# Chunk 5's scores from stacked keys and queries in an mLSTM layer with two gated feed-forward layers

## The chip, the cores and the metric

One core of one Trainium2 chip. The metric is the device time of one execution in microseconds (us), the median of three runs. The profile is of one further execution.

## The reference

Three stages follow each other, all in float32.

```python
# 1: mLSTM attention, B=2, H=8, S=768, D=40; for each t:
m_new = maximum(f[t] + m, i[t])
C = exp(f[t]+m-m_new) * C + exp(i[t]-m_new) * outer(v[t], k[t])
n = exp(f[t]+m-m_new) * n + exp(i[t]-m_new) * k[t]
y[t] = sigmoid(o[t]) * (C @ q[t]) / maximum(abs(n @ q[t]), 1)
# 2: x = y as [1536, 320];  x = (sigmoid(x @ w_gate) * (x @ w_val)) @ w_out     (d_ff = 1536)
# 3:                        x = ((x @ w_a) * (x @ w_b)) @ w_out2                (d_ff = 1536)
```

## The kernel before, in words

**Tiling.** The attention is done in 12 chunks of 128 steps; chunk n is batch n % 2 and time block n // 2. The feed-forward layers work on three groups of 512 tokens (4 chunks) and 12 tiles of 128 hidden columns. One pass of one tile over one group is a unit, and there are 72 units in all. A unit's `up` (line 558) makes 16 matmuls of 512 columns, 8 for the gate and 8 for the value, from the weights' high and low parts, and `down` (L580) makes 12 matmuls of 320 columns.

**Interleaving.** Chunks 0 to 3 come first. Chunk 4 is begun ahead of unit 0, and from there on one chunk goes with three units: `piece(u)` (L79) gives chunk n and step k of unit u. Unit 0 is (4, 1), unit 1 is (4, 2), unit 2 is (5, 0), unit 3 is (5, 1), unit 4 is (5, 2), unit 5 is (6, 0) and so on. On TensorE (L640 to L661) the scores of chunk n stand between the two halves of `up` in the unit with k = 1, and its values behind `down` of the unit before. In the unit with k = 2 the state matmuls stand between the halves, and `turn(n)` (L515), which transposes the chunk's finished output `x_n`, stands ahead of `down(u - 1)`. So whatever holds up a turn holds up all of TensorE's program.

**Scores, two ways.** `scores` (L438) has two forms. Below `STACKED` it is 4 matmuls of float32 keys `k3` against a block-diagonal `q_blk` (L472), and the trace shows each as two instructions. From `STACKED` on it is 8 matmuls, one to a head, of `stack[0]` against `stack[1]` (L463). A stack holds a head's 40 rows three times over in its 120 partitions, as high and low parts in float32r. `load_both` (L297) brings keys (to `k_both`) and queries (to `q_blk[0]`) from DRAM, three times each, in 12 transfers of 120 or 40 KB, 960 KB in all. ScalarE's `part_high` (L689) copies each with a sign by row to the stack, and VectorE's `stack_low` (L933) adds the rest. These stand in the unit with k = 2 ahead of the chunk: on ScalarE ahead of the copy of the turned output and of the two weight tiles' copies (L823 to L836), on VectorE behind `h_low` and ahead of `x_low` (L1052 to L1056).

**Weights.** Each weight tile of 544 KB comes by `load_w(j)` (L334) to a ring of three `w_raw`; ScalarE's `w_high(j)` (L701) makes the high part, GpSimd's `w_low(j)` (L1110) the low part. `load_w(j)` waits until tile j - 3 has been through both. `up(u, 0)` of the first group waits for `w_low` of its tile.

**Other work on the way to a turn.** SyncE's `load_o(4)` (L329) brings chunk 4's output gate. In unit 0 ScalarE's program is `gate(0)`, `w_high(2)`, `open_gate(4)` (L696, the sigmoid of the output gate), `h_high(0)`. VectorE's is `hidden(0)`, `h_low(0)`, then in unit 1 `combine(4)` (L891), `state(4)`, `hidden(1)`. GpSimd's is `decay(4)`, `open_x(4)` (L1077, two multiplications that give `x_n`), `mask(5)`, `w_low(3)`. All these queues run strictly in program order, and the order is written out by hand.

SyncE's program just ahead of the loop, and the guard of its transfers:

```python
load_w(2)
sp.wait_ge(dve_gate, 20)
store_rows(m_row, a_dram, 2, CHUNKS, st_rows)
load_w(3)
load_o(4)
load_w(4)
...
wait(sp, dve_stack, 2 * (n - STACKED))                    # load_both(n)
wait(sp, pe_s, 2 * n if n == STACKED and x else 0)        # x = 1: the queries
```

Of the kernel before, what the change touches and what calls it, by code (L numbers as in the profile page):

```python
# [43 lines left out]
UNITS = 2 * NG * NF  # L44
ALONE = 4
RING = 3
STACKED = 6
LOW = -1.0e30
BIG = 2.0 ** 100
HI, LO = 0, 32  # L50
# [2 lines left out]
def wait(eng, sem, value):  # L53

    if value > 0:
        eng.wait_ge(sem, value)


def set_of(n):

    return n % 2 if n < ALONE else 0
# [17 lines left out]
def piece(u):  # L79

    n, k = divmod(u + 1, 3)
    n += ALONE
    return (n, k) if n < NCH else (None, None)
# [7 lines left out]
def build(nc, f_in, i_in, q_in, kq3_in, vk_in, o_in, w1_in, w2_in, consts_in, bm_in, out):  # L91
    ctx = ExitStack()
    with ctx:
# [172 lines left out]
        def _(sp):  # L266
            def load_rows(n):

                s = set_of(n)
                if n > ALONE:  # L270
                    sp.wait_ge(act_e, 2 * n)
                else:
                    wait(sp, pe_ab, 2 * before(n) + 2)
                if n > ALONE:
                    sp.dma_start(levels[s][:, :],
                                 a_dram[n * HEADS * P:(n + 1) * HEADS * P].partition_broadcast(P)).then_inc(ld_a[s], 16)
                    return
                for at, tile in ((HI, a_hi), (LO, a_lo))[:1 if n < BATCH else 2]:
                    sp.dma_start(arow[s][at:at + 1, :].bitcast(F32), row_source(tile, n)).then_inc(ld_a[s], 16)

            def load_k(n):

                s = set_of(n)
                wait(sp, pe_s, 2 * before(n) + 2)
                sp.dma_start(k3[s][:, :], kq3_in[n, :, 0:3 * P]).then_inc(ld_q[s], 16)

            def load_q(n):

                s = set_of(n)
                if n >= BATCH:  # L290
                    load_k(n)
                for j, k in ((0, 3), (1, 3), (2, 2)):
                    own = slice(j * HD, (j + 1) * HD)
                    sp.dma_start(q_blk[s][own, 3 * j * P:(3 * j + k) * P],
                                 kq3_in[n, own, 3 * P:(3 + k) * P]).then_inc(ld_q[s], 16)

            def load_both(n):  # L297

                wait(sp, dve_stack, 2 * (n - STACKED))
                for x in range(2):  # L300
                    wait(sp, pe_s, 2 * n if n == STACKED and x else 0)
                    for r in range(3):
                        own = both[x][r * HD:(r + 1) * HD, :]
                        sp.dma_start(own[:, 0:6 * P].rearrange("d (j c) -> d j c", j=2),
                                     kq3_in[n, 0:2 * HD, 3 * x * P:3 * (x + 1) * P]
                                     .rearrange("(j d) c -> d j c", j=2)).then_inc(ld_both[x], 16)
                        sp.dma_start(own[:, 6 * P:], kq3_in[n, 2 * HD:, 3 * x * P:(3 * x + 2) * P]
                                     ).then_inc(ld_both[x], 16)

            def load_v(n):  # L310

                s = set_of(n)
                wait(sp, pe_fv, before(n) + 1)
                wait(sp, pe_t, before(n) + 1 if last_with_state(before(n)) else 0)
                sp.dma_start(vk[s][:, :], vk_in[n]).then_inc(ld_v[s], 16)

            def load_scaled(n):

                s = set_of(n)
                wait(sp, pe_f, before(n) - 1)  # L320
                sp.dma_start(q3[s][:, :], kq3_in[n, :, 3 * P:6 * P]).then_inc(ld_i[s], 16)
                rows = i_dram[n * HEADS * P:(n + 1) * HEADS * P].rearrange("(h t) -> h t", t=P)
                for j in range(3):
                    src = rows[j::3, :].unsqueeze(0)
                    k = src.shape[1]
                    sp.dma_start(i_rep[s][j * HD:(j + 1) * HD, 0:k * P].rearrange("d (x t) -> d x t", t=P),
                                 src.to_broadcast([HD, k, P])).then_inc(ld_i[s], 16)

            def load_o(n):  # L329

                wait(sp, pool_x, n if n > ALONE else 0)
                sp.dma_start(osig_b[n % 2][:, :], o_in[:, n * DM:(n + 1) * DM]).then_inc(ld_o[n % 2], 16)

            def load_w(j):  # L334

                wait(sp, act_whi, j - RING + 1)
                wait(sp, pool_wlo, j - RING + 1)
                sp.dma_start(w_raw[j % RING][:, :], (w1_in, w2_in)[j // NF][j % NF]).then_inc(ld_w[j % RING], 16)

            def store_rows(tile, dst, c0, c1, done):  # L340

                sp.dma_start(dst.rearrange("(c r t) -> r c t", r=ROWS, t=P)[:, c0:c1, :],
                             tile[:, c0 * P:c1 * P].rearrange("r (c t) -> r c t", t=P)).then_inc(done, 16)
# [42 lines left out]
            load_w(2)  # L386
            sp.wait_ge(dve_gate, 20)
            store_rows(m_row, a_dram, 2, CHUNKS, st_rows)
            load_w(3)
            load_o(4)  # L390
            load_w(4)
# [2 lines left out]
            for u in range(3 * (NCH - ALONE) - 2):  # L394
                n, k = piece(u)
                if k == 0 and n > ALONE:
                    load_o(n)
                if k == 1 and n + 1 < NCH:
                    load_rows(n + 1)
                    if n + 1 < STACKED:  # L400
                        load_q(n + 1)
                    elif n + 1 == STACKED:
                        load_both(n + 1)
                if k == 0 and STACKED <= n < NCH - 1:
                    load_both(n + 1)
                if k == 2 and n + 1 < NCH:
                    load_scaled(n + 1)
                    load_v(n + 1)
                if u + 5 < NF:
                    load_w(u + 5)  # L410
# [13 lines left out]
        def _(pe):  # L424
# [13 lines left out]
            def scores(n, half):  # L438

                s = set_of(n)  # L440
                if n >= STACKED:
                    wait(pe, dve_stack, 2 * (n - STACKED) + 2)
# [814 lines left out]
```

## Time and profile before

| what | value |
|---|---|
| median of three runs | 467.82 us (467.71 to 467.88) |
| the profiled execution's own time | 467.95 us |
| its span | 466.1 us |
| TensorE busy | 459.0 us |
| VectorE, ScalarE, GpSimd busy | 197.9, 197.5, 114.2 us |
| moved by the transfers | 37.42 MB |

The span is what the profiler saw from the first to the last instruction; the execution's own time holds 1.85 us besides. In the rows below a timeline line gives the start (us from the span's start), the length, the engine, the kernel's line, the operation, what it writes and reads, and in brackets how long the engine stood idle before it and what released it. In the chain of work that ended last a line gives start, length and the work. PE is TensorE, DVE VectorE, ACT ScalarE, POOL GpSimd and SPq the SyncE queue that issues transfers.

### The profile page before, as it was taken

The page shows a single profiled execution, that of the slowest core. Times are in us where ns is not written, and L with a number is a line of the kernel's source. Part 1 is how long each engine was busy: PE and PEld are TensorE (multiplying, and loading weights), DVE is VectorE, ACT ScalarE, POOL GpSimd, SP SyncE. Part 2 cuts the span into 40 slices and gives each one's busy share as a digit, 9 for nine tenths or more (in the row PEclk, how much of TensorE's full clock was granted, in tenths as well). Part 3 has the DMA queues.
Part 4 walks back from the last instruction along what each step waited for, and adds up shares of the span by engine and source line. Part 5 has one row for each costly group of instructions (what it writes and reads, how often), then busy time and mean ns, then how long its engine had stood idle before and what let it go on. Part 6 is the DMA issues. An engine that isn't in the chain of part 4 may idle for free.

```text
span 466.1 us, 6631 instructions
## 1 busy us (share of the span) xinstructions
PE 459.0 (98%) x2527; PEld 403.6 (87%) x2527; DVE 197.9 (42%) x352; ACT 197.5 (42%) x360; POOL 114.2 (25%) x110
## 2 busy tenths in 40 slices
PE   8999999999999999999999999999999999999997
PEld 5888898898989899888888888888888888888886
DVE  8778366746564645334222243222322222322223
ACT  5964838566482836233434452222222222222222
POOL 4488757643213020002445540000000000000000
DMA  5887686352534460000332300000010000100001
GB/s 156 219 271 220 206 248 183 124 155 76 135 110 139 113 203 35 1 2 13 128 99 97 96 1 0 0 2 0 9 49 1 0 1 0 58 0 1 0 1 56
DMA packets 21449, 37.42 MB, mean 80 GB/s; under 512 B 2835, under 2 KB 15670, under 8 KB 21418
## 3 DMA queue, kind: packets, MB, share of 16 engines
q1 hardware_dynamic: 21050, 35.94, 25.4%
q10 hardware_dynamic: 208, 0.71, 0.5%
q8 instruction: 20, 0.33, 0.3%
q0 software_dynamic: 160, 0.35, 0.3%
q14 instruction: 11, 0.09, 0.1%
HBM read 34.91 MB, written 2.04 MB: 79 GB/s over the span
## 4 chain that ended last, share of the span: by engine, by line
PE 86%; DVE 5%; ACT 3%; issue 2%; POOL 2%; DMA 2%; SPq 1%; ACTq 0%; DVEq 0%; POOLq 0%
PE bank L575 53%; PE bank L592 26%; PE bank L497 3%; DMA w_raw<-w_in 1%; ACT pt L680 1%; PE bank L488 1%; PE bank L463 1%; PE bank L553 1%; PE bank L523 1%; DVE h_lo L955 1%; POOL cst L1100 1%; POOL x_n L1085 1%; DVE pt L886 1%; DMA f_row<-f_in 1%; DVE sign L1036 1%
## 5 line engine op out<-in xcount | busy, mean ns | idle before, releaser
L949 DVE TENSOR_TENSOR h_ff<-bank,s_ff 128x512 f32<-128x512 f32 x72 | 49.8, 691 | 173.2 <-PE bank L575 173.0
L575 PE MATMUL bank<-xt,w_hi 128*128 128x512 f32 x360 | 118.7, 395 | 0.0
L744 ACT CAST h_hi<-h_ff 128x512 fp32r<-128x512 f32 x72 | 44.6, 619 | 126.5 <-DVE h_ff L949 123.5
L737 ACT ACTIVATE s_ff<-bank 128x512 f32<-128x512 f32 x72 | 43.1, 598 | 126.0 <-PE bank L575 125.6
L575 PE MATMUL bank<-xt,w_lo 128*128 128x512 f32 x216 | 84.4, 391 | 0.0
L955 DVE TENSOR_TENSOR h_lo<-h_ff,h_hi 128x512 fp32r<-128x512 f32 x72 | 59.6, 828 | 57.3 <-ACT h_hi L744 57.3
L575 PEld LDWEIGHTS bank<-xt,w_hi 128*128 128x128 f32 x360 | 65.5, 188 | 12.0 <-DVE t_st L923 0.4
L575 PE MATMUL bank<-xt,w_hi_mid 128*128 128x512 f32 x180 | 59.2, 394 | 0.0
L575 PE MATMUL bank<-xt,w_hi_end 128*128 128x512 f32 x180 | 59.1, 393 | 0.0
L575 PEld LDWEIGHTS bank<-xt,w_lo 128*128 128x128 f32 x216 | 40.6, 188 | 8.8
L592 PE MATMUL bank<-w_hi,h_hi 128*128 128x320 f32 x144 | 45.3, 314 | 0.2 <-DVE h_lo L955 0.2
L592 PE MATMUL bank<-w_lo,h_hi 128*128 128x320 f32 x144 | 44.4, 308 | 0.0
L592 PE MATMUL bank<-w_hi,h_lo 128*128 128x320 f32 x144 | 44.4, 308 | 0.0
L575 PE MATMUL bank<-xt,w_lo_end 128*128 128x512 f32 x108 | 42.2, 391 | 0.0
L575 PE MATMUL bank<-xt,w_lo_mid 128*128 128x512 f32 x108 | 42.2, 391 | 0.0
L1114 POOL TENSOR_TENSOR w_lo<-w_raw,w_hi 128x1088 fp32r<-128x1088 f32 (+1 forms) x12 | 29.8, 2484 | 45.9 <-ACT w_hi L716 45.9
L575 PEld LDWEIGHTS bank<-xt,w_hi_end 128*128 128x128 f32 x180 | 32.9, 188 | 5.8
L575 PEld LDWEIGHTS bank<-xt,w_hi_mid 128*128 128x128 f32 x180 | 32.8, 188 | 5.7
L592 PEld LDWEIGHTS bank<-w_hi,h_hi 128*128 128x128 f32 x144 | 27.1, 188 | 1.6 <-DVE h_lo L955 0.6
L592 PEld LDWEIGHTS bank<-w_lo,h_hi 128*128 128x128 f32 x144 | 27.1, 188 | 1.2
L592 PEld LDWEIGHTS bank<-w_hi,h_lo 128*128 128x128 f32 x144 | 27.0, 188 | 0.0
L575 PEld LDWEIGHTS bank<-xt,w_lo_mid 128*128 128x128 f32 x108 | 20.3, 188 | 4.4
(125 smaller groups left out, 677.9 us busy)
## 6 DMA issues: line engine op xcount, KB each, us to landing
w_raw<-w_in SPq DMA_DIRECT2D x24, 544.0 KB, 4.0
vk<-vk_in SPq DMA_DIRECT2D x12, 344.0 KB, 3.4
levels<-a_scratch SPq DMA_DIRECT2D x7, 512.0 KB
k_both<-kq_in SPq DMA_DIRECT2D x18, 120.0 KB
q_blk<-kq_in SPq DMA_DIRECT2D x18, 120.0 KB
y<-rows_t SPq DMA_DIRECT2D x12, 160.0 KB, 1.9
q<-kq_in SPq DMA_DIRECT2D x10, 180.0 KB
osig_b<-o_in SPq DMA_DIRECT2D x8, 160.0 KB, 3.0
```

The lines of the kernel that those rows point to most:

```text
L463: mm = pe.matmul(st[:, h * P:(h + 1) * P], stack[0][:, own], stack[1][:, own], start=True, stop=True)
L488: mm = pe.matmul(acc[:, h * VW:(h + k) * VW], q3[s][:, x * P:(x + 1) * P], cst[p][:, h * VW:(h + k) * VW], start=(x == 0), stop=False)
L497: mm = pe.matmul(acc[:, h * VW:(h + 1) * VW], pt[s][:, h * P:(h + 1) * P], vk[s][:, h * VW:(h + 1) * VW], start=(n < BATCH and h == 0), st ...
L523: mm = pe.transpose(tp[:, j * P:(j + 1) * P], x_n[s][:, j * P:(j + 1) * P], ident[:, :])
L553: mm = pe.transpose(tp[:, j * P:(j + 1) * P], rows_t[tb][:, j * P:(j + 1) * P], ident[:, :])
L575: mm = pe.matmul(up_bank(u, gv)[:, :], w_part(low, f, (gv * 3 + kt) * P, P), xt[:, xb * TOK + g * TG:xb * TOK + (g + 1) * TG], start=(j == ...
L592: mm = pe.matmul(OB[tb][:, 0:DM], h[r][:, tb * P:(tb + 1) * P], w_part(low, f, W1C, DM), start=(f == 0 and j == 0), stop=(f == NF - 1 and ...
L737: act.activation(s_ff[u % 2][:, :], up_bank(u, 0)[:, :], ACT.Sigmoid if u < UNITS // 2 else ACT.Copy).then_inc(act_s, 1)
L744: act.copy(h_hi[u % 2][:, :], h_ff[u % 2][:, :]).then_inc(act_h, 1)
L949: dve.tensor_tensor(h_ff[u % 2][:, :], up_bank(u, 1)[:, :], s_ff[u % 2][:, :], ALU.mult).then_inc(dve_h, 1)
L955: dve.tensor_tensor(h_lo[u % 2][:, :], h_ff[u % 2][:, :], h_hi[u % 2][:, :].bitcast(F32), ALU.subtract).then_inc(dve_hlo, 1)
L1114: pool.tensor_tensor(w_part(1, j % NF, at, WC - at), w_raw[j % RING][:, at:], w_part(0, j % NF, at, WC - at).bitcast(F32), ALU.subtract).t ...
```

## The change

`STACKED` goes from 6 to 5, so chunk 5's scores are computed in the stacked form. Its `load_both` no longer stands in the loop; it is issued once ahead of `load_w(3)`. Within unit 1 its two copies (ScalarE) and two sums (VectorE) are new, by the loop's own conditions. In unit 0 the plain loads of chunk 5 (`load_q(5)`, one transfer of keys and three of queries, 340 KB) are gone, and `load_both(6)` moves from unit 3 to unit 2.

```diff
-STACKED = 6
+STACKED = 5
...
             store_rows(m_row, a_dram, 2, CHUNKS, st_rows)
+            load_both(STACKED)
             load_w(3)
             load_o(4)
             load_w(4)
...
                 if k == 1 and n + 1 < NCH:
                     load_rows(n + 1)
-                    if n + 1 < STACKED:
-                        load_q(n + 1)
-                    elif n + 1 == STACKED:
-                        load_both(n + 1)
                 if k == 0 and STACKED <= n < NCH - 1:
                     load_both(n + 1)
```

## Rows read from the trace of the kernel before

**Rows 1.** The page: busy time of TensorE, and VectorE's group of line 955.

```profile
PE 459.0 (98%) x2527; PEld 403.6 (87%) x2527; DVE 197.9 (42%) x352; ACT 197.5 (42%) x360; POOL 114.2 (25%) x110
...
L955 DVE TENSOR_TENSOR h_lo<-h_ff,h_hi 128x512 fp32r<-128x512 f32 x72 | 59.6, 828 | 57.3 <-ACT h_hi L744 57.3
```

**Rows 2.** The waits of TensorE from 30 us to the end: total, times, longest.

```profile
PE bank L523 <- POOL x_n L1085: 1.4, 3, 0.8
```

**Rows 3.** The chain that ended last, 50 to 60 us (unit 3).

```profile
52.35 1.84 PE bank L575 x8
54.20 1.73 PE bank L472 x8
55.93 1.85 PE bank L575 x8
```

**Rows 4.** The same chain, 94 to 101 us (unit 9).

```profile
97.42 0.85 PE bank L463 x8
98.26 1.90 PE bank L575 x8
```

**Rows 5.** Timeline of SyncE's queue ahead of and within unit 0.

```profile
30.54 0.42 SPq L342 DMA_DIRECT2D a_scratch<-m_row  x1
32.62 0.33 SPq L338 DMA_DIRECT2D w_raw<-w_in  x1
32.99 0.43 SPq L332 DMA_DIRECT2D osig_b<-o_in  x1
38.68 0.33 SPq L338 DMA_DIRECT2D w_raw<-w_in  x1
```

**Rows 6.** Timeline of SyncE's queue in unit 5: first issue of load_both(7), and the one behind.

```profile
71.29 0.30 SPq L304 DMA_DIRECT2D k_both<-kq_in  x1
...
75.91 0.35 SPq L338 DMA_DIRECT2D w_raw<-w_in  x1
```

**Rows 7.** The chain that ended last, 70 to 90 us.

```profile
75.91 5.04 DMA w_raw<-w_in
```

**Rows 8.** Tile osig_b, 20 to 95 us: issue to landing of its transfers.

```profile
DMA to landing us min/median/max: 2.3/4.1/6.7
```

**Rows 9.** Busy time by engine, 31 to 36 us, with clock, DMA share, GB/s last.

```profile
31.00:36.00 5.00, 4.98 (x25) 3.83 (x26) 4.13 (x9) 4.15 (x7) 5.00 (x6) 1.00 0.91 319
```

**Rows 10.** Timeline of ScalarE in units 0 and 1.

```profile
37.54 0.47 ACT L699 ACTIVATE osig_b<-osig_b 128x320 f32<-128x320 f32 x1 [0.75 <-DMA osig_b<-o_in]
...
39.26 0.62 ACT L744 CAST h_hi<-h_ff 128x512 fp32r<-128x512 f32 x1 [1.25 <-DVE h_ff L949]
...
45.58 2.11 ACT L716 CAST w_hi<-w_raw 128x1088 fp32r<-128x1088 f32 x2
```

**Rows 11.** Lines 694 and 936: shortest, middle and longest in ns, all six chunks.

```profile
L694 ACT ACTIVATE k_stack<-k_both,sign x6: 1146/1149/1151, 67.6 to 171.9; 120x1024 fp32r<-120x1024 f32 x6
```

```profile
L936 DVE SCALAR_TENSOR_TENSOR k_stack<-k_both,low_rows,k_stack x6: 1284/1285/1286, 68.8 to 173.1; 120x1024 fp32r<-120x1024 f32 x6
```

**Rows 12.** Timeline of VectorE in unit 0.

```profile
36.16 2.47 DVE L1036 TENSOR_SCALAR sign<-low_rows 120x2 f32<-120x2 f32 x1
...
39.91 1.72 DVE L955 TENSOR_TENSOR h_lo<-h_ff,h_hi 128x512 fp32r<-128x512 f32 x1 [0.69 <-ACT h_hi L744]
```

**Rows 13.** Timeline of GpSimd, units 0 to 4.

```profile
35.84 5.24 POOL L1114 TENSOR_TENSOR w_lo<-w_raw,w_hi 128x1088 fp32r<-128x1088 f32 x2
...
43.45 1.12 POOL L1085 TENSOR_TENSOR x_n<-x_raw,osig_b 128x320 f32<-128x320 f32 x1
...
46.77 2.54 POOL L1114 TENSOR_TENSOR w_lo<-w_raw,w_hi 128x1088 fp32r<-128x1088 f32 x1 [0.89 <-ACT w_hi L716]
...
63.66 0.86 POOL L1085 TENSOR_TENSOR x_n<-x_raw,osig_b 128x320 f32<-128x320 f32 x1
```

**Rows 14.** Timeline of TensorE: the turns of chunks 4 and 5.

```profile
44.62 0.55 PE L523 MATMUL bank<-ident,x_n 128*128 128x128 f32 x3 [0.77 <-POOL x_n L1085]
...
66.16 0.49 PE L523 MATMUL bank<-ident,x_n 128*128 128x128 f32 x3
```

## The prediction

> **What bounds the kernel now.** I read the page first. TensorE is busy for 98% of the span, and no other engine for more than 42% [rows 1]. Its waits came next: from 30 us to the end it stands still for its turns alone, 1.4 us in three waits, each for GpSimd's `x_n` [rows 2]. So any TensorE time saved behind 30 us comes off the end, and any lateness of another engine counts only where it reaches TensorE. The timelines then show where the margins are thin. Chunk 4's turn already comes late by 0.77 us [rows 14], so that chain has no slack at all.
>
> **Removed: the plain scores of chunk 5.** In unit 3 the eight plain instructions hold the chain for 1.73 us, with 1.85 us for the half of `up` behind them [rows 3]. In unit 9, of the same make-up, the eight stacked ones take 0.85 us, with 1.90 behind them [rows 4]. The saving is (1.73 + 1.85) - (0.85 + 1.90) = 0.83 us. Nothing hides TensorE, so all of it counts, unless a new stall eats it. `load_q(5)` goes too, four issues in unit 0 behind `load_w(4)`; nothing waited for them, so I take nothing for that.
>
> **Added: 12 issues on SyncE ahead of `load_w(3)`.** In unit 5 the same 12 begin at 71.29 and the issue behind them at 75.91 [rows 6], which is 4.62 us. SyncE is free from 30.54 + 0.42 = 30.96 and idles until 32.62, so part of the block fits in a gap [rows 5]. The queries wait for chunk 4's scores, the last TensorE work ahead of unit 0; they should be through at about the time (33.3) at which the six key issues are, so I price that wait at nothing. Then `load_w(3)` is issued at 30.96 + 4.62 = 35.6 and not 32.62, `load_o(4)` at 36.0 and not 32.99. Both are 3.0 us later. `load_w(4)` waits for GpSimd in any case and goes out at 38.68 [rows 5]: no change.
>
> **Who waits for these two.** Tile 3 is read by ScalarE at 45.58 only [rows 10], and by 41 it has landed: hidden. The gate is another matter. ScalarE's `open_gate(4)` already sat idle 0.75 us for it and began at 37.54, 4.55 us after the issue [rows 5, 10]. Three estimates give its new landing. The same 4.55 from 36.0 gives 40.55. The bytes ahead of it give the same: at 319 GB/s, with the transfers' engines 91% busy in that stretch [rows 9], 960 KB cost 3.0 us. A weight tile issued right behind this very block took 5.04 us to land [rows 7], so tile 3 would land at 40.65 and the gate some 0.4 us behind it, at 41.1. The shortest landing of this tile is 2.3 us and the longest 6.7 [rows 8], so the bounds are 38.3 and 42.7. I take 40.6, where two of the estimates agree.
>
> **What the late gate does.** Behind `open_gate(4)` on ScalarE stands `h_high(0)`, and behind that on VectorE `h_low(0)`, `combine(4)`, and on GpSimd `open_x(4)`, for which the turn waits. `h_high(0)` began at 39.26 [rows 10]. Now it begins at 40.6 + 0.4 = 41.0 and ends at 41.6. `h_low(0)` then starts at 41.65. It took 1.72 us before, from 39.91 to 41.63, beside GpSimd's two weight tiles that ran until 41.08 [rows 12, 13]. Now it starts behind them and takes about the group's mean of 0.83 [rows 1], so it ends at 42.5, later by 0.85. From there to the end of `x_n` at 44.57 [rows 13] the chain is unchanged, perhaps 0.1 shorter for less company. Chunk 4's turn comes 0.75 us later, a stall of 0.77 + 0.75 = 1.5. If the gate lands at 38.3, ScalarE has it before `h_high(0)` could start and nothing is lost; if at 42.7, the turn comes 2.1 us later than in my estimate, so the term lies between 0 and +2.9.
>
> **Moved in unit 1: two copies on ScalarE, two sums on VectorE.** The copies are 1.15 us each and overlap a little, 2.2 us together; the sums are 1.28 each [rows 11]. Their data are in by 39 to 40, well ahead. On ScalarE they stand ahead of `w_high(3)`, which began at 45.58 [rows 10], while `w_low(3)` ended at 46.77 + 2.54 = 49.31 [rows 13] and unit 3 began at 52.35 [rows 3]: a slack of 3.0 us. Against it stand 2.2 us of copies and about 1.2 of lateness that VectorE passes on through `hidden(1)`, while TensorE itself is later by 0.75. That leaves 0.4 us: just hidden. The sums end before `hidden(2)` is due, and `x_low(4)` is not read before the second group.
>
> **Further on in units 2 to 4.** ScalarE stays some 2 us late through the exponentials of chunk 5 and the copies of tiles 5 and 6; GpSimd's low parts of these stand ahead of `decay(5)` and `open_x(5)`. The latter ended at 63.66 + 0.86 = 64.52, with its turn at 66.16 [rows 13, 14], a slack of 1.64. By then TensorE stands at 66.16 - 0.83 + 0.75, about 66.1, and `x_n` is ready at about 66.4 to 66.5. I take a new stall of 0.3 us, between 0 and 0.8. Then the idle of all three engines absorbs the lateness. `load_both(6)` moves to unit 2, where it delays `load_w(7)` and the levels of chunk 6 by some 4 us, against more than that of slack; `load_both(7)` waits for chunk 6's sums as before, so the later stalls [rows 2] remain.
>
> **The sum.** -0.83 + 0.75 + 0.3 = +0.2 us, on the profiled execution's 467.95: 468.15. That execution was 0.13 us above the median of the runs, so against the median it is 468.0. A measurement of this kernel can tell about 0.2%, 0.94 us, from no change.
>
> **One rule of the skill weighed.** What the rows show: `sign`, a 120x2 operation, took 2.47 us, and `h_low(0)` 1.72, each ending just behind a GpSimd weight tile [rows 12, 13]. The Trainium skill (SBUF — State Buffer, "SBUF: two separate sides") says that VectorE and GpSimd share one pair of ports as an exclusive lock for a whole instruction; the trace agrees, by these two durations. By that rule the lateness in unit 2 can grow, which is the second rival below.
>
> **Rival 1: the loads are hidden.** If the gate lands by 39, ScalarE's `h_high(0)` isn't moved and the saving stands alone: 467.82 - 0.83 = 467.0. For it: the shortest landing of 2.3 us. Against it: ScalarE already waited for this transfer with 3 us more to spare. It is still within 0.2%. Chance 0.19, and 0.07 more that a stall shrinks as well and it falls below 466.9.
>
> **Rival 2: slower, through GpSimd's low parts.** `w_low(3)` now falls where VectorE has the added sums and `h_low(2)`, and `w_low(4)` where `h_low(2)` is due. If VectorE must sit out one tile more (2.5 us [rows 13]) or GpSimd one sum more (1.3 us [rows 11]), the slack of 0.4 in front of unit 3 becomes a stall of 0.9 to 2.1, and the turn of chunk 5 slips with it. The time would be 468.0 + 1.3 or so, 469.3 (468.9 to 470.1). It decides as soon as ScalarE's tile 3 copy ends later than about 50.4 (52.35 + 0.75 less 2.54 and a tenth). For it: two thin margins in a row. Against it: in the later chunks, where the same copies and sums stand, TensorE lost little. Chance 0.16. Beside this the gate could land at 42 or later, which gives 469.5 to 470 by the same turn; chance 0.06.
>
> **How the numbers follow.** The forecast (a new stall that about cancels the saving) has 0.52: 467.2 to 468.75. Faster by over 0.2% gets 0.07, slower 0.22, within it 0.71. The range runs from 466.9 to 469.5: the low end is the bare saving, the high end the middle of the slower cases, with about 2 in 10 outside.
>
> **What would show it.** Right: unit 3's scores take 0.85 us; `load_w(3)` is issued near 35.6; ScalarE's idle ahead of `open_gate(4)` grows to near 4 us; chunk 4's turn waits 1.5 us and not 0.77. Wrong: that turn still waits 0.8 us (rival 1), or a wait of `up` for `w_lo` appears ahead of unit 3 or TensorE's wait for chunk 5's turn is over 1 us (rival 2).

## The result and the profile after

| | before | changed |
|---|---|---|
| median | 467.85 us (467.71 to 469.89, 4 runs) | 475.21 us (474.82 to 476.55, 4 runs) |
| profiled execution: own time, span | 467.95, 466.1 us | 476.55, 474.8 us |
| mean granted clock of TensorE | 1.0 | 0.987 |

The ratio is 1.014 (95% interval 1.0104 to 1.0176): 7.4 us slower, where 468.0 (466.9 to 469.5) was forecast. The profiled execution is the longest of the four, 1.3 us above their median. In the changed kernel every line number behind line 400 is 3 lower, so line 575 is now 572.

The waits of TensorE, longest first, in the changed kernel:

```profile
PE bank L520 <- POOL x_n L1082: 7.5, 3, 6.9
```

It is the wait of [rows 2], and it has grown from 1.4 to 7.5 us, 6.9 of it at one place. The chain that ended last, from 36 to 66 us, tells which place and why:

```profile
36.65 0.35 SPq L338
...
37.05 8.86 DMA osig_b<-o_in
...
45.93 0.48 ACT osig_b L696
...
49.45 1.13 POOL x_n L1082
...
50.62 0.90 PE bank L520 x3
51.53 3.20 PE bank L589 x12
54.73 4.63 PE bank L572 x16
59.36 1.76 PE bank L589 x12
61.12 1.84 PE bank L572 x8
62.96 0.85 PE bank L460 x8
63.81 1.90 PE bank L572 x8
```

Chunk 4's output gate is issued at 37.05 and takes 8.86 us to land. ScalarE's sigmoid begins at 45.93 and not 37.54 [rows 10], and chunk 4's turn at 50.62 and not 44.62 [rows 14]. Then look at TensorE's own lengths: the first `down` behind the wait takes 3.20 us, the next one 1.76, for the same 12 matmuls. At the end stand the stacked scores, 0.85 us and not 1.73 [rows 3]. The busy time in stretches of 4 us shows both causes (TensorE's, its loads', VectorE's, ScalarE's and GpSimd's busy time with counts, then the clock, the transfer engines' share, GB/s):

```profile
36.00:40.00 4.00, 4.00 (x31) 3.71 (x30) 3.38 (x3) 1.10 (x1) 4.00 (x3) 1.00 0.91 201
40.00:44.00 4.00, 3.75 (x20) 2.86 (x18) 0.00 (x0) 0.00 (x0) 1.95 (x2) 1.00 1.03 224
44.00:48.00 4.00, 0.00 (x0) 0.00 (x0) 0.99 (x4) 1.47 (x3) 0.00 (x0) 0.81 1.02 375
48.00:52.00 4.00, 1.38 (x6) 1.38 (x7) 3.17 (x6) 1.52 (x2) 2.46 (x3) 0.50 0.49 149
52.00:56.00 4.00, 4.00 (x15) 3.71 (x14) 3.29 (x5) 3.56 (x5) 1.36 (x1) 0.50 0.00 0
56.00:60.00 4.00, 4.00 (x20) 3.37 (x19) 0.60 (x1) 2.39 (x4) 4.00 (x4) 0.91 0.40 135
60.00:64.00 4.00, 4.00 (x26) 3.62 (x25) 1.29 (x3) 3.97 (x10) 1.33 (x1) 1.00 0.75 226
```

From 36 to 44 us the transfer engines are full, yet they bring only 201 and 224 GB/s, against 319 in [rows 9]. And the granted clock, 1.00 until TensorE stopped at about 43.7, is 0.50 from 48 to 56: the lower of its two levels, 1.2 GHz, also for the first matmuls after the wait.

**Where the time went.** The stretch ahead of unit 0 changes from execution to execution (32.4 to 42.6 us in the profiles of this study; in the long ones TensorE's clock is at 0.50 for much of it, also in a variant of the kernel before), so from here on I count from the first matmul of unit 0 (32.88 us in the kernel before, 32.80 in the changed one) to the end of the span.

| stretch (us from unit 0's first matmul) | before | changed | difference |
|---|---|---|---|
| to chunk 4's turn | 11.74 | 17.82 | +6.08 |
| turn to chunk 5's scores | 9.41 | 12.18 | +2.77 |
| scores to the `down` behind them | 3.59 | 2.74 | -0.85 |
| on to the last `down` | 400.20 | 400.23 | +0.03 |
| last `down` to the end | 8.28 | 9.03 | +0.75 |
| sum | 433.22 | 442.00 | +8.78 |

The spans are read to 0.1 us, so the last two rows are good to about 0.05. The +0.75 at the end was no part of any theory. SyncE's wait for the last stores tells it, 1.5 us in the kernel before and 2.2 in the changed one:

```profile
SPq L93 <- DMA y<-rows_t: 1.5, 1, 1.5
```

```profile
SPq L93 <- DMA y<-rows_t: 2.2, 1, 2.2
```

### The profile page after: what moved, and what is told of

It is laid out like the page before. It is cut to its first block, busy times and chain, and to the rows that moved or that the text cites. A ratio compares the mean times of both kernels' runs of the same rounds, so it can differ in the third digit from the quotient of the medians.

```text
span 474.8 us, 6645 instructions
## 1 busy us (share of the span) xinstructions
PE 461.2 (97%) x2527; PEld 405.7 (85%) x2527; DVE 196.6 (41%) x354; ACT 199.1 (42%) x362; POOL 113.7 (24%) x110
## 4 chain that ended last, share of the span: by engine, by line
PE 85%; DMA 3%; DVE 3%; ACT 3%; SPq 2%; issue 2%; POOL 1%; ACTq 0%; DVEq 0%
PE bank L572 52%; PE bank L589 26%; PE bank L494 3%; DMA osig_b<-o_in 2%; DMA w_raw<-w_in 1%; PE bank L460 1%; ACT pt L677 1%; SPq L304 1%; SPq L307 1%; PE bank L485 1%; PE bank L550 1%; PE bank L520 1%; PE bank L508 1%; DMA f_row<-f_in 1%; DVE pt L883 0%
## 5 line engine op out<-in xcount | busy, mean ns | idle before, releaser
L952 DVE TENSOR_TENSOR h_lo<-h_ff,h_hi 128x512 fp32r<-128x512 f32 x72 | 55.3, 768 | 64.3 <-ACT h_hi L741 64.3
```

The lines of the kernel that those rows point to most:

```text
L952: dve.tensor_tensor(h_lo[u % 2][:, :], h_ff[u % 2][:, :], h_hi[u % 2][:, :].bitcast(F32), ALU.subtract).then_inc(dve_hlo, 1)
```

## The experiments

The chips that these ran on scattered more: the kernel before gave 467.3 to 477.5 us, with medians of 468.5 to 469.5. A ratio of whole times then has an interval of some 0.3% either way, so most verdicts rest on the stretches of the profiled executions, counted as above. That is one execution of each kernel, and they differ: the changed kernel took 442.00 us from unit 0 on in one profile and 438.49 in another (e12 below). Where the timed runs say something else than the profile, it is said.

### What stands ahead of the gate

**e1_gate_first:**

```diff
-            load_both(STACKED)
-            load_w(3)
             load_o(4)
+            load_both(STACKED)
+            load_w(3)
             load_w(4)
```

> Chunk 5's 12 transfers stay ahead of weight tile 3, but the output gate's transfer goes ahead of them. Theory A (the 7 us are the gate's late landing and what follows from it): the gate lands by 37.5 us or so, the turn of chunk 4 waits 1 us or less, TensorE's clock stays at full speed, and the time is the kernel before less 0.83 us plus at most 1 us: 467.0 to 468.0. Theory B (the added copies and sums in unit 1, or tile 3 behind 960 KB, are the loss): still over 470, with a wait for w_lo or w_hi ahead of unit 3.

Measured: the gate was no longer waited for, chunk 4's turn came at 11.72 and the clock stayed at 1.0. At the last `down` the kernel was ahead of the kernel before by 0.86 us, and at the end of the span by 0.08: 433.14 against 433.22. Ratio 1.0018 (0.9991 to 1.0046). Its turn wait, of the whole execution:

```profile
PE bank L520 <- POOL x_n L1082: 1.4, 3, 0.7
```

Theory B falls here. The copies, the sums and a tile 3 behind 960 KB are all still in this kernel, and in this execution not one of them stops TensorE.

**e2_block_behind:**

```diff
-            load_both(STACKED)
             load_w(3)
             load_o(4)
+            load_both(STACKED)
             load_w(4)
```

> The 12 transfers go behind tile 3 and the gate and ahead of tile 4, into the stretch in which the transfers stood still in the kernel before (36 to 39 us). Theory A: nothing that is waited for stands behind them; the gate lands at 37.5 as before, tile 4 and the levels are not late, and the bare saving is left: 467.0, between 466.8 and 467.5. Theory B (copies and sums cost): 468 to 469 by a stall in units 1 to 4.

Measured: turn at 11.74 with a wait of 0.77, as in [rows 14]; 0.79 us ahead from unit 3 to the last `down`, and 433.14 at the end. Ratio 1.0009 (0.9982 to 1.0036). The saving is real and is carried through all of the feed-forward work; 0.72 us of it go at the very end (below).

**e3_keys_ahead** (`load_both` in two halves: the keys where the change has it, the queries behind `load_o(4)`):

```diff
-            load_both(STACKED)
+            load_both(STACKED, (0,))
             load_w(3)
             load_o(4)
+            load_both(STACKED, (1,))
```

> Half the dose: the six transfers of the keys (480 KB) stay ahead of tile 3 and the gate, the six of the queries go behind them. If the lateness grows with what stands ahead, the gate lands between the kernel before (37.5) and the changed one (45.9): near 40 if it is the issues and bytes alone, and the turn of chunk 4 waits 1 to 2 us with the clock at full speed, 467.5 to 468.5. If the clock falls even so, 470 or more.

Measured: the gate took 6.9 us from issue to use. In the profiled execution it was issued early against TensorE's work (unit 0 began at 37.16), and the turn waited only 0.89 us. Behind it the clock stayed at 1.00, and from unit 0 on it took 433.14 us, no more than the kernel before. Over the timed runs the median was 472.76, ratio 1.0059 (1.0029 to 1.009), with a clock of 0.978 to 0.996 in each of the eight runs above 471. That half the dose stops TensorE at the turn in many of these is likely but not shown: the profiled execution is one of the eight, and its low clock lay ahead of unit 0 (0.50 from 30 to 34 us). What is shown is that the gate's landing grows with what stands ahead of it, and by more than I priced.

**e6_issues_only** (12 transfers of 4 bytes in place of the block, the real block behind the gate):

```diff
-            load_both(STACKED)
+            for i in range(12):
+                sp.dma_start(tiny[:, i:i + 1], kq3_in[5, 0:1, i:i + 1]).then_inc(ld_extra, 16)
             load_w(3)
             load_o(4)
+            load_both(STACKED)
```

> Twelve transfers of 4 bytes each stand ahead of tile 3 and the gate, chunk 5's real ones behind the gate. It is the lateness of the issue alone, some 4 to 5 us of queue without bytes: by my working the gate lands near 40.5 and the turn waits 1.5 us; 467.8 to 468.5. If small issues cost more than that it is seen as SyncE's gaps.

Measured: issued 2.1 us later against unit 0, the gate was used 3.6 us after its issue, and the turn waited 0.74 us. The waits in that execution:

```profile
PE bank L525 <- POOL x_n L1087: 1.5, 3, 0.7
```

So the late issue by itself costs nothing at the turn; without the block's bytes the gate even lands sooner behind its issue than the 4.55 us of the kernel before. The timed median was 469.83, ratio 1.0007 (0.9981 to 1.0032). From unit 0 on it took 434.34 us, 1.2 more than e2_block_behind; 0.8 of that builds up at 0.02 us a unit from unit 27 on, for which see the end of the experiments.

**e5_whole_width** (in `load_both`, for chunk 5 only; chunk 5's scores come from other columns, so that part of the computation is changed):

```diff
+                    if n == STACKED:
+                        sp.dma_start(both[x][:, 0:6 * P], kq3_in[n, :, :]).then_inc(ld_both[x], 48)
+                        sp.dma_start(both[x][:, 6 * P:], kq3_in[n, :, 0:2 * P]).then_inc(ld_both[x], 48)
+                        continue
```

> The changed kernel with the same 960 KB at the same place in 4 transfers over all 120 partitions (3072 and 1024 bytes a row) and not in 12 over 40 partitions; they bring other columns than the stacks need, so chunk 5's scores are computed from wrong rows and the output of that chunk and all after it differs. If the form or number of the transfers is what is slow: tile 3 and the gate are issued at 32.6 and land near 38 to 41, time 467 to 469. If it is the bytes: the gate still lands at 43 or later and the time stays over 472.

Measured: in the profiled execution the gate, issued 1.5 us after unit 0's start, was used 8.5 us later, and the turn waited 3.69 us. From unit 0 on it took 438.48 us, as much as the changed kernel in e12. So 960 KB ahead of the gate can hold up the turn in this form too. But the timed median was 470.78, ratio 1.0026 (0.9989 to 1.0063), between my two cases (467 to 469, over 472). Six of the ten runs took 468.3 to 471.4 us with a clock of 0.999 or 1.0; the changed kernel never came below 472.35 in its ten runs, and the profiled execution was the third slowest here. So the form or the number of the transfers matters as well: wider and fewer ones give back most of the loss in most executions. How much of that is the earlier issue and how much the form, no run separates.

The shares in the changed kernel hint at the form. While the block is being issued, the transfer engines are 0.58 to 0.71 busy from 33 to 37 us. In unit 5 of the kernel before, where the same block is nearly alone, it is much the same. The changed kernel's line comes first, then three of the kernel before:

```profile
34.00:35.00 1.00, 0.99 (x5) 0.50 (x4) 0.90 (x3) 0.32 (x2) 1.00 (x1) 1.00 0.58 197
```

```profile
72.00:73.00 1.00, 1.00 (x9) 1.00 (x8) 0.26 (x1) 0.98 (x3) 1.00 (x1) 1.00 0.45 122
73.00:74.00 1.00, 1.00 (x8) 0.96 (x7) 0.44 (x1) 0.99 (x2) 1.00 (x2) 1.00 0.61 168
74.00:75.00 1.00, 1.00 (x6) 0.82 (x5) 0.00 (x0) 1.00 (x4) 1.00 (x2) 1.00 0.66 170
```

The packets' start and end times in the traces say the same: of this block mostly 10 packets are under way at once, of the weight tiles around 34 us in the kernel before 16, and of e5's wider transfers 14 or 15. So the transfers over 40 partitions seem to use some 10 of the 16 engines, and the tile's and the gate's packets on these would stand behind 960 KB spread over 10. That it is this which delays the gate wasn't tested.

**e7_hold_behind** (`sp.wait_ge(ld_o[0], 16)` ahead of `load_w(4)`):

> The changed kernel, with everything behind the gate's transfer (tile 4, the levels, tile 5, chunk 5's other loads) held back until the gate has landed. If transfers issued later take the gate's share (the gate took 8.9 us from issue to landing, and the rate was 190 to 246 GB/s while the transfers' engines were full), it lands by 41 to 42 and the time falls to 470 or below. If it is what stands ahead of it that is slow, it lands at 44 to 46 all the same and the time is 475 or more, since levels and tile 4 now come late too.

Measured: with nothing issued behind it until it had landed, the gate still took 8.1 us, the turn waited 5.0 and the execution took 439.05 us from unit 0 on. The timed median was 474.56, ratio 1.0116 (1.0075 to 1.0157), like the changed kernel's. It is what stands ahead that is slow, not what comes behind: in the profiles with the changed order and nothing held back the gate took 8.9, 6.6 (e12) and 6.0 us (e8), so 8.1 is within their spread and no gain. This kernel also shows how long the block keeps the transfer engines. Here are its rates in single microseconds, when only the block, tile 3 and the gate were left:

```profile
38.00:39.00 1.00, 1.00 (x11) 1.00 (x11) 1.00 (x2) 0.00 (x0) 1.00 (x2) 1.00 1.09 243
39.00:40.00 1.00, 1.00 (x8) 0.92 (x8) 0.39 (x1) 0.00 (x0) 1.00 (x1) 1.00 1.08 176
40.00:41.00 1.00, 1.00 (x6) 0.83 (x5) 0.00 (x0) 0.00 (x0) 1.00 (x1) 1.00 0.74 143
```

Summed over its single microseconds from 31 to 44, the share makes 9.9 us of full transfer engines. In the kernel before the same sum from 31 to 37, with nearly everything but the block, makes 4.8. So the block's 960 KB added 5.1 us of full engines, about 190 GB/s, and not the 3.0 us at 319 GB/s of the prediction. Its own packets make 3.9 us of this; the other packets beside them got slower as well. The Trainium skill (DMA: Bandwidth & Descriptors, "Anatomy of one DMA — SWDGE (gpsimd) path") gives a fixed 2.0 us and 436 GB/s for a transfer that GpSimd issues, by which an estimate for 960 KB is 2.3 us of moving. These transfers are issued by SyncE, so the page's figure was not made for them; the measurement is more than twice as long, and it decides.

### The clock

**e8_pe_kept_busy:**

```diff
+                if u == 1:
+                    pe.wait_ge(dve_y, ALONE)
+                    for _ in range(24):
+                        pe.matmul(OB[0][:, :], w_part(0, 0, 0, P), xt[:, 0:TG], start=True, stop=True)
                 if k == 2:
                     turn(n)
```

> The changed kernel, with 24 matmuls of 512 columns (5.5 us at full clock) added ahead of the turn of chunk 4, within the wait of 6.9 us; their result is not used. Their work costs nothing if the wait is there anyway. Theory C (about 2.7 us of the loss are the clock, which the rows show at half after the wait): with TensorE at work the granted clock stays at 1.0 through units 1 and 2 and the time falls by 2 to 3 us against the changed kernel, to 472 to 473. If the clock is not the matter, no change or up to 1 us slower.

The chain that ended last in that kernel, 50 to 70 us; line 649 is the added work, ahead of the turn:

```profile
52.80 5.46 PE bank L649 x24
58.27 0.33 PE bank L520 x3
58.60 1.76 PE bank L589 x12
60.36 3.65 PE bank L572 x16
```

The 12 matmuls of `down` take 1.76 us and not 3.20, and the 16 of `up` 3.65 and not 4.63. From the turn to chunk 5's scores it is 9.35 us, against 12.18 in the changed kernel and 9.41 before. The clock was 1.00 from unit 0 on. So the 2.77 us are the clock's, and TensorE standing still is their cause. The Trainium skill (TensorE: Matmul & The Clock Gate, "Part 1: The HAM clock gate") has the slow level as the state of rest, which activity releases; the trace agrees, with 0.50 behind the wait and 1.00 where the wait was filled. One stretch of this trace doesn't fit it so simply. The execution was a long one, 481.21 us, because unit 0 began at 42.13 us only; ahead of it the clock was at 0.50 from 20 to 40 us although TensorE was busy:

```profile
28.00:32.00 4.00, 4.00 (x21) 4.00 (x21) 0.82 (x4) 0.24 (x1) 0.00 (x0) 0.50 0.65 208
```

As a remedy the filling is worth less than 2.77 us. `x_n` was ready at 55.68, and the added work held the turn up until 58.1; from unit 0 on it took 437.34 us, against 438.49 and 442.00 in the two profiles of the changed kernel. The timed runs don't tell them apart: a median of 473.78 and a ratio of 1.0092 (1.006 to 1.0124), against 475.91 and 1.0112 (1.0057 to 1.0168) for the changed kernel alone (next).

**e12_change_again** (the changed kernel as it is):

> The changed kernel once more, on this chip and beside the kernel before on it: the gate lands 8 to 9 us after its issue, the turn of chunk 4 waits 5 to 7 us, the clock falls to half behind that wait, and the time is 473 to 477, 6 to 8 above the kernel before.

Measured: 475.91 us, ratio 1.0112 (1.0057 to 1.0168). In its profiled execution the gate took 6.6 us, less than I expected, the turn waited 3.48 us, below the 5 to 7 expected, and from the turn to the scores it took 12.03 us: a wait of 3.5 us cost about as much clock (2.6 us) as one of 6.9 (2.8). The other kernels with a long wait had 2.4 us (e5, a wait of 3.7) and 1.5 us (e7, 5.0), so the price doesn't go by the wait's length. The stretches behind the wait:

```profile
44.00:46.00 2.00, 0.00 (x0) 0.00 (x0) 1.83 (x6) 0.00 (x0) 0.61 (x2) 0.94 1.04 336
46.00:50.00 4.00, 3.17 (x13) 3.17 (x14) 3.31 (x5) 3.31 (x5) 1.84 (x2) 0.50 0.41 104
50.00:54.00 4.00, 4.00 (x15) 3.37 (x15) 1.51 (x3) 2.13 (x3) 3.15 (x2) 0.67 0.00 0
```

### The end of the execution

In every kernel with chunk 5 stacked the profile counts one packet more on the queue that loads instructions, 12 and not 11, and one falls among the last stores. The queues of e2_block_behind in its last 8 us:

```profile
q1 hardware_dynamic: 576, 0.66, 23.5%
q14 instruction: 1, 0.01, 0.5%
```

The kernel before has only the first of these two lines there. But the count is of the span alone. From 466.2 to 472 us, behind its last instruction, the kernel before has this:

```profile
q14 instruction: 1, 0.01, 0.4%
```

So in the kernels before and changed it is the same number of loads. The last one came 1.8 us behind the end in the kernel before and comes 2.1 to 2.6 us ahead of the end in those with chunk 5 stacked. The expectations below go by the count within the span. Eight kernels sought whose program brings it.

| kernel | edit | loads on q14 within the span | one among the last stores | last wait, us |
|---|---|---|---|---|
| e9_fewer_sp | e2, SyncE without `wait(sp, act_whi, j - RING + 1)` | 12 | yes | 2.3 |
| e13_shorter_act | e2, ScalarE without 13 waits for `dve_sign` | 12 | yes | 2.1 |
| e14_shorter_dve | e2, VectorE without 10 waits for `pe_fv` in `product` | 12 | yes | 2.3 |
| e15_both_shorter | the two above together | 12 | yes | 2.1 |
| e10_longer_sp | before, 29 more waits on SyncE | 12 | no | 1.5 |
| e11_shorter_before | before, SyncE without the same waits as e9 | 11 | no | 1.5 |
| e16_longer_act | before, 16 one-element copies on ScalarE in unit 60 | 12 | no | 1.5 |
| e17_longer_dve | before, 16 one-element copies on VectorE in unit 60 | 11 | no | 1.5 |

> The 12 transfers behind tile 3 and the gate, as in e2_block_behind, and SyncE's 24 waits for w_high taken out, which the waits for w_low imply. In every kernel with chunk 5 stacked the last stores took 0.6 to 0.8 us longer to be seen as landed (SyncE waits 2.1 to 2.3 us for them and not 1.5), and 12 and not 11 instruction loads are counted on queue 14. Theory D (SyncE's longer program sets it): with the waits gone 11 loads are counted, the last wait is 1.5 again and from unit 0's start to the end it is 432.4 us, 0.8 below the kernel before. Theory E (chance of the chip or of the run): 2.1 to 2.3 still, and 433.1.

> The kernel before with 29 more waits on SyncE ahead of the loop, each for what has already come. Theory D: a twelfth instruction load, the last wait 2.1 to 2.3 us, and 433.9 us from unit 0's start to the end against 433.2. Theory E: as before, 1.5 and 433.2, or either by chance.

> The kernel before without the 24 waits for w_high on SyncE. Control for e9_fewer_sp: theories D and E both expect no change from the kernel before if the last wait is 1.5 us there; 433.2 from unit 0's start to the end. If 1.5 and 2.2 depend on the chip, it shows 2.2 here.

Theory D falls by both ends: taking SyncE's waits out left 2.3 us, and 29 more in the kernel before left 1.5. (The twelfth load of e10 is one at 0.2 us that falls just ahead of the span elsewhere; its last one still comes behind the end.) e11 shows that 1.5 doesn't hang on the chip. The ratios of the timed runs were 1.0014 (0.9979 to 1.0049) for e9, 1.0015 (0.9976 to 1.0054) for e10 and 0.9997 (0.9961 to 1.0034) for e11.

e9's profiled execution took 434.42 us, more than expected, and shows a thin place of this order of the loads. GpSimd stood still for the levels of chunk 5, which land late when the block is ahead of them, and the low part of tile 3 behind them came late for unit 3. GpSimd's rows, and the wait of TensorE's weight load:

```profile
48.28 1.11 POOL L1103 TENSOR_SCALAR_AFFINE_SELECT levels<-levels 128x1024 f32<-128x1024 f32 x1 [4.24 <-DMA levels<-a_scratch]
49.36 2.52 POOL L1110 TENSOR_TENSOR w_lo<-w_raw,w_hi 128x1088 fp32r<-128x1088 f32 x1
```

```profile
51.94 0.30 PEld L571 LDWEIGHTS bank<-xt,w_hi 128*128 128x128 f32 x2 [0.38 <-POOL w_lo L1110]
```

Chunk 5's scores began at 21.51 there and at 21.40 in e13, against 21.15 before: 0.25 to 0.36 us of the saving are lost in such executions, and next to none in the profiled ones of e1, e2, e14 and e15 (21.11 to 21.19). The larger part of e9's loss comes later, at chunk 6's turn: it waits 1.18 us there for `x_n`, against 0.46 in e2 and 0.47 in the kernel before. e15 waits 0.79 at the same place.

> The 12 transfers behind tile 3 and the gate, and 13 of ScalarE's 14 waits for the signs taken out (the first implies them). In all kernels with chunk 5 stacked an instruction load on queue 14 falls between the last stores (at 465 us), and none does in the kernel before, with or without a longer SyncE program. Theory F (ScalarE's program, longer by two copies and their waits, calls for one more block): that load is gone, 11 are counted, the last wait is 1.5 us and unit 0's start to the end is 432.4. If it is VectorE's program, no change: 12 loads, 2.1 to 2.3, 433.1.

> The same transfers, and on VectorE 10 waits for the values' matmuls taken out, which the waits for the exponentials imply. Theory G (VectorE's program, longer by two sums and their waits, calls for one more block at the end): 11 loads, a last wait of 1.5 us, 432.4 from unit 0's start to the end. If it is ScalarE's, no change: 12, 2.1 to 2.3, 433.1.

> Both sets of waits taken out. If either F or G holds: 11 loads, 1.5 us and 432.4, which is the bare saving of 0.8 us against the kernel before; the median is 0.8 us below it, within what this chip's scatter of 2 us lets be seen. If neither holds: 433.1 and no difference that can be measured.

F and G weren't borne out: 12 loads and 2.1 to 2.3 us in all three, 433.3 to 433.5 from unit 0 on. The ratios were 0.9987 (0.9955 to 1.002), 0.997 (0.9943 to 0.9997) and 0.9991 (0.9965 to 1.0018). At the last `down` e14 was 0.84 us ahead of the kernel before and e15 0.49.

> The kernel before with 16 copies of one element added on ScalarE in unit 60, where it is idle most of the time; nothing reads them. Theory F (ScalarE's longer program brings the load at the end): a twelfth load on queue 14, among the last stores, SyncE's last wait 2.1 to 2.3 us and not 1.5, and 433.9 us from unit 0's start to the end. Otherwise 11 loads, 1.5 us and 433.2.

> The same on VectorE: 16 copies of one element in unit 60. Theory G (VectorE's longer program brings it): a twelfth load on queue 14 among the last stores, 2.1 to 2.3 us, 433.9. Otherwise 11, 1.5 and 433.2.

In e16 the last load moved from behind the end to 452.0 us, 15 us ahead of the end and clear of the stores, and the last wait stays at 1.5. In e17 it stayed 1.8 us behind the end. That points to ScalarE's program as the one that this load serves, although 13 waits fewer on ScalarE (e13) left it among the stores. The load among the stores and the later landing go together in every kernel here, but that the one causes the other stays open.

Both kernels, timed once each, took 0.9 us more up to the last `down`, and not through the copies: nothing jumps at unit 60. The difference grows by 0.02 us a unit from about unit 26 on, as in e6. These three are the kernels in which a small tile, `tiny`, and a semaphore were added; in none of the others does it grow like this. Which of the two does it, and how, wasn't tried, and the edits were less neutral than they look. TensorE's own program, which also changes with the form of the scores, wasn't tried.

## Why the prediction was wrong

- **What bounds the kernel, and where a lateness would count:** right, but for 0.2 us that TensorE also waits for `h_lo`. Chunk 4's turn, behind the output gate, was the place.
- **The saving, 0.83 us:** right. It measured 0.85 at its place, and 0.79 to 0.86 at the last `down` of e1 and e2.
- **"Who waits for these two", the gate's landing at 40.6:** this is the step that failed. It landed at 45.9, beyond my bound of 42.7. The term that was mis-sized is the time from the gate's issue to its landing: 8.9 us, and 8.1, 6.6 and 6.0 in the profiles of e7, e12 and e8, not 4.55. The 960 KB were priced at 319 GB/s, the rate of a stretch with mostly weight tiles in it; they added 5.1 us of full engines (e7). And none of the three estimates had this queue in it. The 4.55 us was the landing without the block. The 5.04 us was behind the block, but the engines were idle as it began (a share of 0.04 from 71 to 72 us), where in the changed kernel they were full (1.06 from 32 to 33). The bound of 6.7 us was the longest landing in a kernel that never has such a block ahead of a gate, so it was no bound. A second term was off in the profiled execution alone: the issue behind the block went out at 36.65 and not 35.6, since three of the 12 issues took 0.6 us and not 0.34. In e7, e8 and e12 the block took 4.7 us, as forecast.
- **The stall of +0.75 us (0 to +2.9):** +6.08, by that step alone; +2.71 in the profile of e12.
- **The clock:** missing altogether. A wait of 0.77 us left it at 1.0 in the kernel before, and I never asked what a wait several times as long would do: +2.77 us.
- **Moved in unit 1, "just hidden":** hidden, by e1 and e2, and as thin as I put it: in e9 and e13, where the levels came late, tile 3's low part held unit 3 up by 0.25 to 0.36 us, which is the sign that I gave for rival 2, at a smaller price. The stall of 0.3 us at chunk 5's turn didn't come either: e2 is 0.79 us ahead at that turn.
- **Rival 2, through GpSimd's low parts:** it didn't happen in the changed kernel. TensorE is itself so late there that the low part of tile 3 is ready long before unit 3.
- **The chances:** the case of a late gate had 0.06, with a price of 469.5 to 470. It should have been the main rival, since a transfer that the kernel already waits for was being moved behind nearly a megabyte.
- **The end:** 0.75 us that nothing in the diff touches.

## What to carry to other kernels

Before a block of transfers goes ahead of others on a queue, find the first one behind it that is already waited for, and let that one go first: here moving one line turned 7.4 us of loss into none that could be measured. Price bytes by the rate in a full stretch of the same kind of transfers, not by the best rate in sight, and take a landing from a queue as deep as the new one will be. Look at the count of instruction loads beyond the span before calling one of them new, and don't take an added tile for free. When a wait of TensorE grows from under 1 to several us, add the clock's part to it: here 1.5 to 2.8 us, for waits of 3.5 to 6.9.

## What the runs showed of the hardware

- 960 KB in packets of 1.0 and 1.5 KB, in 12 transfers of 40 partitions, added 5.1 us of full transfer engines beside a weight tile and a gate (about 190 GB/s, e7). Nearly alone, in unit 5 of the kernel before, such a block kept the engines 0.45 to 0.66 busy while it was issued, with mostly 10 of its packets under way at once. The landing behind them took 6.0 to 8.9 us in four profiles, and 8.5 in one of the same bytes in 4 transfers of 120 partitions, whose timed median was still 4 to 5 us lower.
- TensorE's granted clock was 0.50 behind waits of 3.5, 3.7, 5.0 and 6.9 us and 1.00 behind waits of 0.8, and stayed at 1.00 where matmuls of no use filled the wait.
- The final stores landed 0.6 to 0.8 us later in every kernel of this study with chunk 5 stacked, and in each an instruction load fell among them that otherwise came behind the end. Whether it is the cause is open.
- In the three kernels with one small tile and a semaphore more, TensorE's work took 0.02 us a unit longer, 0.9 us in all (e16, e17; e6 alike).
